# Squared-relu attention with all its matmuls in 64-row halves of the array

## The chip, the core and the metric

The kernel runs on one core of a Trainium2 chip. The metric is the time of the device in microseconds (us), as the median over runs of the whole program. The profile is of one execution more, taken by the hardware profiler.

## What is computed

```
scores = z @ z.T / S                       # per batch: S = 3072, 64 columns of z
attn   = maximum(scores, 0) ** 2
x      = u * (attn @ v)                    # D = 256; 8 batches, 24576 rows in all
logits = x @ w_gate                        # 8 experts; softmax; argmax picks one
# the first 768 rows (capacity) of each expert, in order of the rows:
out[i] = gate[i] * (maximum(x[i] @ w1[e], 0) @ w2[e])   # F = 1024; other rows are 0
```

All inputs are float32. Rows that come after an expert is full give zero, so the kernel stops the attention as soon as all eight experts are full.

## The kernel before

**Tiles.** A group is 384 rows of x (three tiles of 128), eight groups a batch. Keys come in 24 chunks of 128, two chunks a double (PAIRS = 12 doubles a group). Float32 values are split in two float16 parts, high and low; products high by high, high by low and low by high are summed in PSUM. zP holds the high part of one half of the keys on partitions 0 to 63 and the low part on 64 to 127 (the other way round for the batch's second half), zQ the same with the halves crossed. One matmul of zP by zP has high by high and low by low, one of zP by zQ the two mixed terms: scores() gives two matmuls of 384 columns for each of the two chunks (L640, L641).

**A double.** TensorE: scores of double c+3 (LEAD), then the values of double c: weigh() issues for each of three tiles and two chunks three matmuls of 256 columns (L676 high by high v, L678 high by low v, L680 low by high v), all summed over 128 keys, into one accumulator a tile (o_part). ScalarE: relu in place in PSUM (do_relu, L462), square with a scale into `attn` in SBUF (do_square, L466). VectorE: a float16 copy attn_hi (do_hi, L941) and the rest attn_lo (do_lo, L947). There are four score banks, two for even and two for odd doubles; `scores(K)` wait until the square of K-2 is done. Values wait for `lo_done`.

**Banks.** O has two banks (three tiles of 256 columns), Sc four, M two: the logits in one, the counts in the other.

**Between groups.** gate_x, at VectorE's step c=11 and before that step's do_hi, multiplies O by the factor of the batch and by u in one operation (L988 for tiles 0 and 1, L992 for tile 2). TensorE's first values of the next group wait for it (evac_done). ScalarE, at c=0, sums absolute values of the result (L503, three times), from which VectorE works out a scale; ScalarE writes high parts at c=1 (L508), VectorE low parts at its c=0 (L1041); SyncE transposes rows by DMA. TensorE does the logits (L717, 12 matmuls of 16 columns) behind tile 2 of c=3 and the counts (L725, L729, 4 matmuls) behind tile 1 of c=4. VectorE routes at its c=3 (L1086 to L1124), all of it between do_lo of the sixth double and do_hi of the seventh; GpSimd scatters the rows to their experts' places.

**Steps beside these.** The engines' programs are the same loop over groups with fixed places for side work: in the last four groups of a batch the split of the next batch's z and v (ScalarE c=6 to 9, VectorE c=7 to 9, among it z_lo_across, a copy to the other half of the partitions, L911), in groups 1 and 2 of a batch the sums of absolute v on ScalarE (L438), four a group. After double END_AT every engine reads whether all experts are full (load_end) and if so leaves. Then the experts' two layers run, in 16 rounds.

**Order.** All engines but TensorE's weight loads go strictly in the order of their programs. wait_apart is a wait on a value that is held in a register, with an increment of a spare semaphore.

## Time and profile before

| | |
|---|---|
| median of 3 runs | 867.1 us (867.08 to 867.22) |
| the profiled execution's span | 865.3 us |
| TensorE busy | 853.5 us (99%) |
| VectorE busy | 632.4 us (73%) |
| ScalarE busy | 574.7 us (66%) |
| GpSimd busy | 123.2 us (14%) |
| attention's last matmul, experts' first | 609.09 us, 609.80 us |
| granted clock of TensorE | full in the whole span |

The median is 1.8 us above the span; what lies between is around the first and the last instruction. Matmuls are pipelined and their ends are modelled: what one costs in a stream is read from start to start. A line is that of the source, L12 line 12. "<-" behind an idle time names what ended it. PE is TensorE's matmuls, PEld its weight loads, DVE VectorE, ACT ScalarE, POOL GpSimd.

### The profile page before, as it was taken

What the parts mean: (1) busy time and instruction counts of PE and PEld (TensorE: products, weight loads), DVE (VectorE), ACT (ScalarE), POOL (GpSimd) and SP (SyncE); (2) the same over time, 40 slices, a digit from 0 to 9 for tenths busy, and PEclk for the clock granted to TensorE, in tenths of its full rate; (3) what the DMA queues carried; (4) which work ended last, traced back from release to release, by engine and by line L of the source; (5) the groups of instructions that cost most, each with busy time, mean ns of one, the idle gap of its engine ahead of it and who ended that gap; (6) DMA issues with size and microseconds to landing.
All of it is one profiled execution on the core that took longest, in us unless ns stands there. A gap on an engine that the chain in (4) does not pass through costs nothing.

```text
span 865.3 us, 22736 instructions
## 1 busy us (share of the span) xinstructions
PE 853.5 (99%) x7258; PEld 683.9 (79%) x7259; DVE 632.4 (73%) x1380; ACT 574.7 (66%) x874; POOL 123.2 (14%) x121
## 2 busy tenths in 40 slices
PE   6999999999999999999999999999999999999997
PEld 5888888888888888888888888888777777777776
DVE  7976777988889878887888798687464655565531
ACT  7978786868778779777778777678434434435422
POOL 1001102101101110110110110110112121211212
PEclk9999999999999999999999999999999999999999
DMA  7922343343312633312313313731625325415101
GB/s 274 372 70 94 87 129 136 100 135 117 118 46 97 240 108 97 115 49 92 115 50 98 107 53 108 264 82 40 145 65 171 102 80 158 142 46 152 55 18 36
DMA packets 104277, 98.62 MB, mean 114 GB/s; under 512 B 67149, under 2 KB 91802, under 8 KB 103232
## 3 DMA queue, kind: packets, MB, share of 16 engines
q1 hardware_dynamic: 99360, 85.71, 32.1%
q0 software_dynamic: 4896, 12.64, 4.0%
q8 instruction: 12, 0.20, 0.1%
q14 instruction: 9, 0.07, 0.0%
HBM read 40.03 MB, written 44.93 MB: 98 GB/s over the span
## 4 chain that ended last, share of the span: by engine, by line
PE 97%; DVE 2%; issue 1%; POOL 0%; ACT 0%; POOLq 0%; DVEq 0%; ACTq 0%
PE O L676 17%; PE O L678 17%; PE O L680 17%; PE Sc L786 14%; PE Sc L640 8%; PE Sc L641 8%; PE O L809 3%; PE O L813 3%; PE O L811 3%; PE M L809 2%; PE M L813 2%; PE M L811 2%; PE M L717 1%; PE M L615 0%; DVE zQ L904 0%
## 5 line engine op out<-in xcount | busy, mean ns | idle before, releaser
L676 PE MATMUL O<-vS,attn_hi 128*128 128x256 f16 x1332 | 363.0, 273 | 0.3 <-DVE vS L930 0.3
L680 PE MATMUL O<-vS,attn_lo 128*128 128x256 f16 x1332 | 363.0, 273 | 0.0
L678 PE MATMUL O<-vS,attn_hi 128*128 128x256 f16 x1332 | 363.0, 273 | 0.0
L462 ACT ACTIVATE Sc<-Sc 128x768 f32<-128x768 f32 x224 | 178.0, 795 | 86.3 <-PE Sc L641 78.4
L947 DVE TENSOR_TENSOR attn_lo<-attn,attn_hi 128x768 f16<-128x768 f32 x223 | 213.7, 958 | 7.7
L466 ACT ACTIVATE attn<-Sc 128x768 f32<-128x768 f32 x224 | 181.7, 811 | 7.1
L676 PEld LDWEIGHTS O<-vS,attn_hi 128*128 128x128 f16 x1332 | 130.2, 98 | 27.2 <-issue 0.4
L678 PEld LDWEIGHTS O<-vS,attn_hi 128*128 128x128 f16 x1332 | 130.3, 98 | 26.6
L640 PE MATMUL Sc<-zP 128*128 (+1 forms) x450 | 146.4, 326 | 2.1 <-DVE zP L911 1.3
L641 PE MATMUL Sc<-zQ,zP 128*128 (+1 forms) x450 | 146.4, 326 | 0.0
L941 DVE CAST attn_hi<-attn 128x768 f16<-128x768 f32 x223 | 123.7, 555 | 27.4 <-ACT attn L466 26.0
L680 PEld LDWEIGHTS O<-vS,attn_lo 128*128 128x128 f16 x1332 | 130.3, 98 | 15.1
L1251 DVE SCALAR_TENSOR_TENSOR rawv<-Sc,rawv 128x768 f16<-128x768 f32 x63 | 60.1, 956 | 110.1 <-ACT rawv L571 110.1
L380 POOL DMA_INDIRECT disp<-xrow,slot x54 | 68.2, 1263 | 486.8 <-DVE slot L1123 453.2
L571 ACT ACTIVATE rawv<-Sc 128x768 f16<-128x768 f32 x63 | 51.1, 811 | 100.8 <-PE Sc L786 99.7
L786 PE MATMUL Sc<-vS,w1h 128*128 128x384 f16 x384 | 78.1, 326 | 0.0
L809 PE MATMUL O<-w2s,rawv 128*128 128x256 f16 x256 | 69.8, 273 | 0.0
L813 PE MATMUL O<-w2s,rawv 128*128 128x256 f16 x256 | 69.8, 273 | 0.0
L811 PE MATMUL O<-w2s,rawv 128*128 128x256 f16 x256 | 69.8, 273 | 0.0
L415 POOL DMA_INDIRECT out<-attn,vS x48 | 47.0, 980 | 113.6 <-ACT attn L583 99.9
L640 PEld LDWEIGHTS Sc<-zP 128*128 128x128 f16 (+1 forms) x450 | 43.9, 98 | 20.4 <-DVE zQ L925 1.5
L641 PEld LDWEIGHTS Sc<-zQ,zP 128*128 128x128 f16 (+1 forms) x450 | 44.0, 98 | 17.1
(155 smaller groups left out, 912.4 us busy)
## 6 DMA issues: line engine op xcount, KB each, us to landing
out<-empty SPq DMA_DIRECT2D x16, 1536.0 KB, 6.3
wraw<-in_moe_w SPq DMA_DIRECT2D x16, 1024.0 KB, 7.0
rawv<-in_v SPq DMA_DIRECT2D x14, 768.0 KB, 8.5
ubuf<-in_u SPq DMA_DIRECT2D x19, 384.0 KB, 3.1
disp<-vS SPq DMA_DIRECT2D x8, 774.0 KB, 9.1
rawz<-in_z SPq DMA_DIRECT2D x3, 768.0 KB, 6.0
xT<-xrow SPq DMA_TRANSPOSE x54, 2.4
disp<-xrow,slot POOLq DMA_INDIRECT x54, 2.8
```

Of the source, the lines that this page charges most:

```text
L462: act.activation(pair, pair, ACT.Relu).then_inc(s["relu_done"], 1)
L466: act.activation(attn[:, c % BUFS, :, :], Sp[:, 2 * (c % 2):2 * (c % 2) + 2, 0:GROUP], ACT.Square, scale=ROOT_C).then_inc(s["square_done"], 1)
L640: nc.tensor.matmul(to, keys, zP[:, bass.ds(qb, GROUP)], start=True, stop=False)
L641: ins = nc.tensor.matmul(to, keys, zQ[:, bass.ds(qb, GROUP)], start=False, stop=True)
L676: nc.tensor.matmul(o_part(t), hi, v[:, 0:D], start=c == 0 and j == 0 and t % 2 == 0, stop=False, skip_group_check=True)
L678: nc.tensor.matmul(o_part(t), hi, v[:, D:2 * D], start=False, stop=False, skip_group_check=True)
L680: ins = nc.tensor.matmul(o_part(t), lo, v[:, 0:D], start=False, stop=c == PAIRS - 1 and j == 1, skip_group_check=True)
L786: ins = nc.tensor.matmul(Sp[:, 2 * (p % 2) + fi, 0:GROUP], w[par][:, m, f * P:(f + 1) * P], xt[k][:, x + m, :], start=(at == 0), stop=(at ...
L809: nc.tensor.matmul(y_part(t), hi, w2s[:, par, f, 0:D], start=f == 0, stop=False, skip_group_check=True)
L811: nc.tensor.matmul(y_part(t), hi, w2s[:, par, f, D:2 * D], start=False, stop=False, skip_group_check=True)
L941: dve.tensor_copy(attn_hi[:, b, :, :].rearrange("p j n -> p (j n)"), attn[:, b, :, :].rearrange("p j n -> p (j n)")).then_inc(s["hi_done"], 1)
L947: dve.tensor_tensor(attn_lo[:, b, :, :], attn[:, b, :, :], attn_hi[:, b, :, :], ALU.subtract).then_inc(s["lo_done"], 1)
```

## The change

Every matmul of the attention phase, the logits and counts too, becomes two: one on partitions 0 to 63 of both operands, one on 64 to 127, issued one after the other and writing to different banks (helper `half`).

- **Scores.** In zP and zQ the high and the low part of a chunk's keys stand on different halves of the partitions. Three terms (high by high, high by low, low by high), each a pair: half 0 does chunk 0 of the double, half 1 chunk 1. Low by low is left out.
- **Values.** The same three matmuls as before, each in two halves of 64 keys, into two sets of banks: O has four banks. M is gone; logits and counts use score banks 2 and 3 (`beside`), and in the loop all scores use banks 0 and 1 (`score_banks`). The norms of the next batch go there too.
- **Relu** goes from PSUM into `attn`, square works in place there. `scores(K)` wait for the relu of K-1.
- **Joining the two sums.** ScalarE copies the second half's banks, scaled, into `lower` (in the memory of xT), VectorE adds the first half's, scaled (evac_done), and multiplies by u in another operation (`gated`). gate_x now comes after do_lo of step c=11. The values of the last two doubles are reordered (TURNS) so that tiles 0 and 1 end earlier. Logits and counts are summed over the halves by VectorE.
- **Queries** are copied by GpSimd into fixed buffers (q_now for the running group, q_next and k_next for the first doubles of the next); it also does z_lo_across.
- **Places.** Logits behind c=3, counts behind c=4 (all tiles), END_AT from 5 to 6, steps of norms and scales later, several small buffers shared.

The diff, cut to its core (smaller memory for tables and renamings are left out):

```diff
-        Oa = ps("O", [P, 2, 512], F32)
+        Os = ps("O", [P, 4, 512], F32)
         Sp = ps("Sc", [P, 4, 512], F32)
-        Mp = ps("M", [P, 2, 512], F32)
-
-        def o_part(t):
-            return Oa[:, t // 2, (t % 2) * D:(t % 2 + 1) * D]
-
-        M = [Mp[:, m, :] for m in range(2)]
+
+        def half(r):
+            return slice(64 * r, 64 * r + 64)
+
+        def o_part(r, t):
+            return Os[:, 2 * r + t // 2, (t % 2) * D:(t % 2 + 1) * D]
+
+        def beside(r, at, columns):
+            return Sp[:, 2 + r, at:at + columns]
+
+        both_counts = Sp[:, 2:4, COUNTS_FROM:COUNTS_FROM + (TILES + 1) * E].rearrange("p r n -> p n r")
+        both_norms = Sp[:, 2:4, 0:GROUP]
+
+        def score_banks(K):
+            return K % 2 if isinstance(K, int) else 0
...
+            def queries(to, m, ready):
+
+                at = (m & 15) * GROUP
+                for q, z16 in zip(to, (zP, zQ)):
+                    pool.tensor_copy(q[:, :], z16[:, bass.ds(at, GROUP)]).then_inc(s[ready], 1)
+
+            def keys(m):
+
+                at = (m & 8) * (S // 8)
+                for k, z16 in zip(k_next, (zP, zQ)):
+                    pool.tensor_copy(k[:, :], z16[:, bass.ds(at, SLICE * P)]).then_inc(s["k_next_ready"], 4)
+
             def body(n, end):
                 g = n & 7
                 if isinstance(n, int):
+                    pool.wait_ge(s["khi_ready"], 2)
+                    pool.wait_ge(s["klo_ready"], 2)
+                    queries(q_now, 1, "q_now_ready")
+                    keys(0)
 
                     pool.wait_ge(s["disp_filled"], 16 * (E * capacity // P // FILL_ROWS))
                     pool.sem_inc(s["row_free"], 1)
                     return
+                wait_apart(pool, s["scores_ready"], n * PAIRS + LEAD)
+                for key in ("khi_ready", "klo_ready"):
+                    wait_apart(pool, s[key], ((n + 1) & 126) + 2)
+                queries(q_next, n + 1, "q_next_ready")
+                only_if(pool, g == 7, lambda: keys(n + 1))
...
+                def keys_low_across():
+
+                    wait_apart(pool, s["q_next_ready"], n * 2)
+                    wait_apart(pool, s["k_next_ready"], ((n + 1) & 120) + 8)
+                    wait_apart(pool, s["zlo_ready"], (n & 120) + g * 2 + 2)
+                    cols = bass.ds(((n + 8) & 8) * (S // 8) + (g & 3) * (SLICE * P), SLICE * P)
+                    with pool.If(g < 6):
+                        pool.tensor_copy(zP[half(1), cols], zQ[half(0), cols]).then_inc(s["klo_ready"], 2)
+                    with pool.Else():
+                        pool.tensor_copy(zQ[half(0), cols], zP[half(1), cols]).then_inc(s["klo_ready"], 2)
+                    wait_apart(pool, s["klo_ready"], (n & 120) + g * 2 + 2)
+
                 def rest():
+                    only_if(pool, g > 3, keys_low_across)
                     only_if(pool, g == 3, reduce_maxes)
                     only_if(pool, n == 7, lambda: all_w(0))
                     only_if(pool, n == 12, lambda: all_w(1))
+                    wait_apart(pool, s["scores_ready"], n * PAIRS + PAIRS)
+                    queries(q_now, n + 1, "q_now_ready")
...
-                pair = Sp[:, 2 * (c % 2):2 * (c % 2) + 2, 0:GROUP]
-                act.activation(pair, pair, ACT.Relu).then_inc(s["relu_done"], 1)
+                at = 2 * score_banks(K)
+                act.activation(attn[:, c % BUFS, :, :], Sp[:, at:at + 2, 0:GROUP], ACT.Relu).then_inc(s["relu_done"], 1)
 
             def do_square(K, c):
                 act.wait_ge(s["relu_done"], K + 1)
-                act.activation(attn[:, c % BUFS, :, :], Sp[:, 2 * (c % 2):2 * (c % 2) + 2, 0:GROUP], ACT.Square,
-                               scale=ROOT_C).then_inc(s["square_done"], 1)
+                act.activation(attn[:, c % BUFS, :, :], attn[:, c % BUFS, :, :], ACT.Square, scale=ROOT_C
+                               ).then_inc(s["square_done"], 1)
...
+                        if not peeled and c == LOWER_AT:
+                            wait_apart(act, s["fcur_ready"], ((n - 1) & 120) + 8)
+                            act.wait_ge(s["o_ready"], n * 2 - 1)
+                            act.activation(lower[:, 0:2, :].rearrange("p t d -> p (t d)"), Os[:, 2, :], ACT.Copy,
+                                           scale=fcur[:, 0:1]).then_inc(s["lower_ready"], 1)
+                            act.wait_ge(s["o_ready"], n * 2)
+                            act.activation(lower[:, 2, :], Os[:, 3, 0:D], ACT.Copy,
+                                           scale=fcur[:, 0:1]).then_inc(s["lower_ready"], 1)
                         if not peeled and c == L1_AT:
                             for t in range(TILES):
-                                act.wait_ge(s["evac_done"], n * 2 - 1 + t // 2)
+                                act.wait_ge(s["gated"], n * 2 - 1 + t // 2)
...
-                if not (isinstance(K, int) and K < 2):
-                    if par is None:
-                        wait_apart(pe, s["square_done"], K - 1)
-                    else:
-                        pe.wait_ge(s["square_done"], K - 1)
-                qb = (n & 15) * GROUP
-                for j in range(2):
-                    at = (2 * c + j) * P
-                    kb = (n & 8) * (S // 8) + at if par is None else par * S + at
-                    keys, to = zP[:, bass.ds(kb, P)], Sp[:, 2 * (c % 2) + j, 0:GROUP]
-                    nc.tensor.matmul(to, keys, zP[:, bass.ds(qb, GROUP)], start=True, stop=False)
-                    ins = nc.tensor.matmul(to, keys, zQ[:, bass.ds(qb, GROUP)], start=False, stop=True)
+                if not isinstance(K, int):
+                    wait_apart(pe, s["relu_done"], K)
+                elif K >= 2:
+                    pe.wait_ge(s["relu_done"], K - 1)
+
+                def key_cols(z16, k_first, r):
+                    at = (2 * c + r) * P
+                    return k_first[half(r), at:at + P] if par is None else z16[half(r), par * S + at:par * S + at + P]
+
+                def query_cols(z16, q_first, q_rest, r):
+                    if isinstance(n, int):
+                        return z16[half(r), n * GROUP:(n + 1) * GROUP]
+                    return (q_first if par is None else q_rest)[half(r), :]
+
+                high_keys, low_keys = (
+                    [key_cols((zP, zQ)[x], k_next[x], r) for x, r in ((h, 0), (1 - h, 1))] for h in range(2))
+                high_queries, low_queries = (
+                    [query_cols((zP, zQ)[x], q_next[x], q_now[x], r) for x, r in ((h, 0), (1 - h, 1))] for h in range(2))
+                terms = ((high_keys, high_queries), (high_keys, low_queries), (low_keys, high_queries))
+                for at, (keys, queries) in enumerate(terms):
+                    for r in range(2):
+                        ins = nc.tensor.matmul(Sp[:, 2 * score_banks(K) + r, 0:GROUP], keys[r], queries[r],
+                                               start=at == 0, stop=at == len(terms) - 1)
...
-                        hi, lo = (a[:, c % BUFS, j, t * P:(t + 1) * P] for a in (attn_hi, attn_lo))
-                        v = vS[:, par * CHUNK + 2 * c + j, :]
-
-                        nc.tensor.matmul(o_part(t), hi, v[:, 0:D], start=c == 0 and j == 0 and t % 2 == 0,
-                                         stop=False, skip_group_check=True)
-                        nc.tensor.matmul(o_part(t), hi, v[:, D:2 * D], start=False, stop=False,
-                                         skip_group_check=True)
-                        ins = nc.tensor.matmul(o_part(t), lo, v[:, 0:D], start=False,
-                                               stop=c == PAIRS - 1 and j == 1, skip_group_check=True)
+                        first, last = c == 0 and j == 0 and t % 2 == 0, c == PAIRS - 1 and j == 1
+                        for at, (weights, low_values) in enumerate(((attn_hi, 0), (attn_hi, 1), (attn_lo, 0))):
+                            for r in range(2):
+                                ins = nc.tensor.matmul(
+                                    o_part(r, t), weights[half(r), c % BUFS, j, t * P:(t + 1) * P],
+                                    vS[half(r), par * CHUNK + 2 * c + j, low_values * D:(low_values + 1) * D],
+                                    start=first and at == 0, stop=last and at == 2, skip_group_check=True)
...
+                            if not peeled and c == 0:
+                                wait_apart(pe, s["q_now_ready"], n * 2)
...
+                                    wait_apart(pe, s["q_next_ready"], n * 2)
+                                    wait_apart(pe, s["k_next_ready"], ((n + 1) & 120) + 8)
                             scores(K0 + c + LEAD, n + 1, c + LEAD - PAIRS, 0 if peeled else None)
 
-                        pe.wait_ge(s["lo_done"], K0 + c + 1)
+                        wait_apart(pe, s["lo_done"], K0 + c + 1)
                         if peeled:
                             pe.wait_ge(s["split_ready"], (2 * c + 1) // UNIT + 1)
-                        for t in range(TILES):
+                        for of, t in TURNS.get(c, [(c, t) for t in range(TILES)]):
                             if c == 0 and not peeled and t != 1:
 
-                                pe.wait_ge(s["evac_done"], n * 2 - 1 + t // 2)
-                            ins = weigh(c, t)
-                            if c == PAIRS - 1 and t:
+                                wait_apart(pe, s["evac_done"], n * 2 - 1 + t // 2)
+                            ins = weigh(of, t)
+                            if of == PAIRS - 1 and t:
                                 ins.then_inc(s["o_ready"], 1)
...
+                        if not peeled and c == LOGITS_AT:
...
+                            for k in range(TILES):
+                                for at, (h, m) in enumerate((h, m) for h in range(2) for m in range(DC)):
+                                    for r in range(2):
+                                        ins = nc.tensor.matmul(beside(r, k * 2 * E, 2 * E),
+                                                               xT[half(r), k, h * DC + m, :], wgs[half(r), m, :],
+                                                               start=at == 0, stop=at == 2 * DC - 1,
...
+                        if not peeled and c == COUNTS_AT:
+                            wait_apart(pe, s["onehot_ready"], n)
+                            for r in range(2):
+                                nc.tensor.matmul(beside(r, COUNTS_FROM, (TILES + 1) * E), before[half(r), :],
+                                                 onehot[half(r), :, :].rearrange("p t e -> p (t e)"),
+                                                 start=True, stop=False, skip_group_check=True)
+                            for k in range(TILES):
+                                for r in range(2):
+                                    ins = nc.tensor.matmul(
+                                        beside(r, COUNTS_FROM + (k + 1) * E, (TILES - k) * E), ones[half(r), :],
+                                        onehot[half(r), k:k + 1, :].to_broadcast([64, TILES - k, E]),
+                                        start=False, stop=k == TILES - 1, skip_group_check=True)
+                            ins.then_inc(s["counts_ready"], 1)
...
+                for k, tiles in enumerate((slice(0, 2), slice(2, 3))):
+                    dve.wait_ge(s["lower_ready"], n * 2 - 1 + k)
+                    dve.scalar_tensor_tensor(out=lower[:, tiles, :].rearrange("p t d -> p (t d)"),
+                                             in0=Os[:, 0, :] if k == 0 else Os[:, 1, 0:D], scalar=fcur[:, 0:1],
+                                             in1=lower[:, tiles, :].rearrange("p t d -> p (t d)"),
+                                             op0=ALU.mult, op1=ALU.add).then_inc(s["evac_done"], 1)
+                    dve.wait_ge(s["evac_done"], n * 2 - 1 + k)
+                    dve.tensor_tensor(ubuf[:, tiles, :], lower[:, tiles, :], ubuf[:, tiles, :], ALU.mult
+                                      ).then_inc(s["gated"], 1)
...
-                        if c == PAIRS - 1:
-
-                            gate_x(n + 1)
                         do_hi(K0 + c + 2, c + 2)
                         do_lo(K0 + c + 2, c + 2)
+                        if c == PAIRS - 1:
+                            gate_x(n + 1)
...
-                            counts = M[1][:, 0:TILES * E].rearrange("p (t e) -> p t e", t=TILES)
+                            route(dve.tensor_reduce(csum[:, :], both_counts, AX.X, ALU.add))
+                            counts = csum[:, 0:TILES * E].rearrange("p (t e) -> p t e", t=TILES)
...
+TURNS = {PAIRS - 2: [(PAIRS - 2, 0), (PAIRS - 2, 1)],
+         PAIRS - 1: [(PAIRS - 1, 0), (PAIRS - 1, 1), (PAIRS - 2, 2), (PAIRS - 1, 2)]}
...
-LOGITS_AT = (3, 2)
-COUNTS_AT = (4, 1)
+LOGITS_AT = 3
+COUNTS_AT = 4
...
-END_AT = 5
+END_AT = 6
```

## Rows read from the trace of the kernel before

**Rows 1.** The page: busy us, share of the span and instructions of each engine
```profile
PE 853.5 (99%) x7258; PEld 683.9 (79%) x7259; DVE 632.4 (73%) x1380; ACT 574.7 (66%) x874; POOL 123.2 (14%) x121
```

**Rows 2.** The stretch view of one group's length: busy us of each engine
```profile
56.70:88.57 31.87, 31.87 (x283) 26.09 (x281) 23.91 (x59) 25.37 (x43) 3.77 (x3) 1.00 0.29 89
```

**Rows 3.** The page's groups of instructions: busy us, mean ns of one | idle before
```profile
L676 PE MATMUL O<-vS,attn_hi 128*128 128x256 f16 x1332 | 363.0, 273 | 0.3 <-DVE vS L930 0.3
```

**Rows 4.** The timeline at a boundary: start us, us, engine, line
```profile
400.05 0.33 PE L641 MATMUL Sc<-zQ,zP 128*128 x1
...
400.21 0.27 PE L676 MATMUL O<-vS,attn_hi 128*128 128x256 f16 x1
400.21 0.10 PEld L678 LDWEIGHTS O<-vS,attn_hi 128*128 128x128 f16 x1
...
402.17 0.33 PE L640 MATMUL Sc<-zP 128*128 x1
...
402.82 0.27 PE L676 MATMUL O<-vS,attn_hi 128*128 128x256 f16 x1
```

**Rows 5.** The timeline of TensorE at the start
```profile
13.79 2.40 PE L647 MATMUL O<-ones,identh 128*128 128x128 f16 x40
```

**Rows 6.** The timeline of TensorE around logits and counts of the same group
```profile
412.63 0.45 PE L717 MATMUL M<-wgs,xT 128*128 128x16 f16 x12
412.94 0.32 PE L640 MATMUL Sc<-zP 128*128 x1
...
414.89 0.18 PE L725 MATMUL M<-onehot,before 128*128 128x32 f16 x1
...
415.00 0.27 PE L676 MATMUL O<-vS,attn_hi 128*128 128x256 f16 x1
```

**Rows 7.** The timeline of ScalarE behind the same boundary
```profile
400.41 0.80 ACT L462 ACTIVATE Sc<-Sc 128x768 f32<-128x768 f32 x1 [0.98 <-PE Sc L641]
401.23 0.81 ACT L466 ACTIVATE attn<-Sc 128x768 f32<-128x768 f32 x1
402.50 0.42 ACT L503 ACTIVATE xrow<-ubuf 128x256 f16<-128x256 f32 x1 [0.46 <-DVE ubuf L988]
...
403.72 0.79 ACT L462 ACTIVATE Sc<-Sc 128x768 f32<-128x768 f32 x1
...
406.44 0.80 ACT L462 ACTIVATE Sc<-Sc 128x768 f32<-128x768 f32 x1
```

**Rows 8.** The groups of VectorE and ScalarE by form
```profile
L947 DVE TENSOR_TENSOR attn_lo<-attn,attn_hi 128x768 f16<-128x768 f32 x223 | 213.7, 958 | 7.7
...
L992 DVE SCALAR_TENSOR_TENSOR ubuf<-O,fcur,ubuf 128x256 f32<-128x256 f32 x18 | 8.5, 474 | 0.0
...
L571 ACT ACTIVATE rawv<-Sc 128x768 f16<-128x768 f32 x63 | 51.1, 811 | 100.8 <-PE Sc L786 99.7
...
L583 ACT ACTIVATE attn<-O,fac 128x256 f32<-128x256 f32 x32 | 15.1, 473 | 18.4 <-PE O L813 18.4
...
L587 ACT ACTIVATE rawv<-Sc 128x384 f16<-128x384 f32 x1 | 0.5, 491 | 4.4 <-PE Sc L786 4.4
```

**Rows 9.** The timeline of VectorE in the same group
```profile
401.72 0.75 DVE L988 SCALAR_TENSOR_TENSOR ubuf<-O,fcur,ubuf 128x512 f32<-128x512 f32 x1 [2.45 <-PE O L680]
...
413.12 0.21 DVE L1086 TENSOR_REDUCE logit<-M 128x24 f32<-128x48 f32 x1 [0.61 <-PE M L717]
...
415.18 0.16 DVE L1112 TENSOR_TENSOR base<-base,M 128x8 f32<-128x8 f32 x1
...
416.57 0.55 DVE L941 CAST attn_hi<-attn 128x768 f16<-128x768 f32 x1
```

**Rows 10.** The timeline of ScalarE in group 1, with sums of v
```profile
72.28 0.80 ACT L462 ACTIVATE Sc<-Sc 128x768 f32<-128x768 f32 x1 [0.34 <-ACT xT L438]
...
75.50 0.80 ACT L462 ACTIVATE Sc<-Sc 128x768 f32<-128x768 f32 x1 [0.61 <-ACT xT L438]
```

**Rows 11.** The groups of GpSimd by form
```profile
L364 POOL MEMSET vS<- 128x1542 f32 x1 | 1.4, 1383 | 0.3 <-POOLq L1348 0.3
```

## What the change is predicted to do

> **What bounds the kernel now.** I read the page's busy times first, then one group in the stretch view, then the timelines. TensorE is busy 853.5 of 865.3 us [rows 1], and what it waits for lies at the start. So the change is worth what it takes off TensorE's stream, less what it makes TensorE wait. A group lasts 31.87 us; in it VectorE is busy 23.9 us and ScalarE 25.4 us [rows 2]. Neither is the bound on average, but both work in strict order, so what counts is which wait ends last at each place. 1332 matmuls at L676 are 222 doubles of six [rows 3]: the flat group 0, seventeen full ones and six doubles of group 18, with 18 boundaries and 18 routings. The pace inside a double: four score matmuls from 402.17 to 402.82, 0.163 us each; eighteen value matmuls from 400.21 to 402.17, 0.109 each; 2.61 us in all [rows 4]. The durations 0.33 and 0.27 beside them are modelled ends, not occupancy.
>
> **Scores.** Two matmuls a key chunk, four a double, become three pairs of half matmuls. If the two of a pair run together, a double's scores cost 3 x 0.163 = 0.49 in place of 0.65. Values stay at 18 x 0.109 = 1.96, now as 18 pairs. A double falls to 2.45 us: 222 x 0.163 = **-36.2 us**. This rests on a pair costing what one matmul costs. Bounds: 40 matmuls of 128 columns take 2.40 us, the tail of the last (0.23 less its own step) included, so 0.0556 each [rows 5]; against 0.109 at 256 columns that is 0.0533 per 128 columns and 0.0023 fixed. If the other half hides the fixed part, 21 x 222 x 0.0023 = 10.7 us go besides; if both halves' parts stand one behind the other, 10.7 us come on top. I take the middle, since nothing in the trace speaks for either end. The second bound is the sequencer, which must hand over a load and a matmul every 0.054 us: the trace shows 0.0556 kept up over 40 [rows 5] and 0.026 for twelve in a row [rows 6]; the middle lies between these too.
>
> The trace has the load for L678 starting at 400.21 together with the matmul of L676, on the same rows of the array [rows 4]. The Trainium skill (TensorE: Matmul & The Clock Gate, The mechanism) says that a load overlaps matmuls in flight only when its row group differs; by that rule each half would stand still for its own next load, by the row it does not. The same section's span model adds about 4 ns for the second tile of a pair; by that, an estimate, 21 x 222 x 4 ns = 19 us would come on top of the sum.
>
> **Small matmuls.** Logits go from 12 to 24; twelve took 412.63 to 412.94, so +0.31. Counts go from 4 to 8; four took 414.89 to 415.00, so +0.11 [rows 6]. They lie on TensorE and nothing hides them: 18 x 0.42 = **+7.6 us** (nothing, if the halves' loads run side by side; this pace looks like one of instructions, so I take the full price). END_AT 6 instead of 5 gives a seventh double of group 18: **+2.5 us**. Fixed query buffers, the closing matmuls, norms and start-up change by tenths: nothing. The last phase is not touched.
>
> **The boundary.** Times from V, the start of the values of c=11 (400.21 before). The last score matmul began at 400.05 and ended at V+0.17, relu began at V+0.20, square 0.82 after it [rows 4, 7]. With TURNS, tiles 0 and 1 of the old group end after twelve pairs, V + 11 x 0.109 + 0.27 = V+1.47. ScalarE is still in its square then. (Relu into SBUF and square out of it keep their length: 768 columns from PSUM to SBUF took 0.811 [rows 8].) Its new copy of the lower half's sum starts at V+1.78. A scaled copy of 256 columns took 0.473; 384 columns more of one operation took 0.811 - 0.491 = 0.32 [rows 8], so 256 more make 0.69: V+2.47. VectorE's fused operation of 512 columns took 0.75 [rows 9], to V+3.25. TensorE wants the bank at V + 24 x 0.109 + 0.49 = V+3.11 and restarts about 0.1 after the signal (a load's recorded length [rows 4]): **0.24 lost**.
> VectorE then multiplies by u, now an operation of its own: 768 columns at L947 took 0.958; 256 columns are 0.751 - 0.474 = 0.28 [rows 8, 9], so 512 make 0.68, to V+3.96. The second bank takes 0.47 and 0.41 more, less what neighbours overlap: V+4.82. ScalarE's last absolute sum waits for this (the three took 402.50 to 403.72, 0.40 each [rows 7]), so its relu of the next double starts at V+5.25 and ends at V+6.05. Here stands the new wait: in the loop all scores use one pair of banks, and scores(K) wait for relu(K-1), where they waited for square(K-2). TensorE wants c=1's scores at V+3.35+1.96 = V+5.31 and starts them at V+6.17: **0.86 lost**. The 36 value matmuls of c=1, whose inputs are long there, are queued behind that wait. Relu, square and three row copies took 2.72 (403.72 to 406.44 [rows 7]), 0.03 more with square from SBUF: the next relu runs from V+8.00 to V+8.82; TensorE wants c=2's scores at V+8.62 and goes on at V+8.94: **0.32 lost**. Then ScalarE has caught up. 1.42 us a boundary, 18 times: **+25.6 us**. Bounds: nothing, if each of the scaled durations is short; 1.9 each, if a copy on GpSimd holds VectorE up as well.
>
> **The routing.** L is the start of the logits (412.63). VectorE read them at L+0.49 and was ready for the counts at L+2.55 (415.18) [rows 6, 9]; now L+0.80 and L+2.86. But the counts move from behind tile 1 to behind all of c=4: L + 0.62 + 2.45 + 0.22 and a tail of 0.17, L+3.46. The new addition over the halves takes 0.24, the old steps 1.39 (415.18 to 416.57 [rows 9]), so the cast of the seventh double starts at L+5.1 and its attn_lo, 0.58 and 0.96 later, ends at L+6.63. TensorE wants it in c=6 at L + 0.64 + 2.45 + 0.22 + 2.45 + 0.49 = L+6.25 and starts at L+6.75: 0.5 x 18 = **+9.0 us**. Bounds: nothing (it had 0.75 us to spare before) to 1 us each.
>
> **The sums of v.** In five groups ScalarE has one of these in each of c=6 to 9, and relu then follows relu by 3.2 us (72.28 to 75.50) [rows 10], against TensorE's 2.45. Relu(K-1) may be late by 1.96 - 0.17 - 0.85 - 0.1 = 0.84 us. The first two are covered by that and by the stall of c=6, the last two lose about 0.47 each: 5 x 0.95 = **+4.8 us**. Bounds nothing to 8.
>
> **GpSimd.** It gets four copies of 384 columns a group, and in four groups of a batch the crossing of the low keys, which VectorE did. q_now is wanted 2.4 us behind a boundary, and the keys cross near the end of the group before. The only plain row of its speed is a fill of 1542 elements in 1.38 us [rows 11]: 0.35 us a copy, 0.7 for the crossing. Several times that is still hidden; past about five times TensorE would wait at every boundary. I put nothing, and 0 to 9 us (0.5 a group) in the range for VectorE being held up.
>
> **Sum.** -36.2 + 7.6 + 2.5 + 25.6 + 9.0 + 4.8 = +13.3, a span of 878.6 from 865.3. The median of the runs stands 1.8 above that span: **880 us**.
>
> **Rivals.**
> (a) Faster: the stalls are mostly covered. The chain at the boundary has eight links, four of them scaled from other shapes. With none of the 39.4 us lost it is 841, with half 861, likeliest 850; it decides below 24 us of stalls. For it: the removed matmuls lay on the bounding engine, and a hidden fixed part would give 10.7. Against: ScalarE's order is strict, and the new wait is for its latest relu. Chance 0.28.
> (b) The forecast, 869 to 890: 0.48.
> (c) Slower still: a pair pays both fixed parts or the sequencer's 0.0556, 10 us, and GpSimd's copies cost up to 9: 890 to 902. 0.14.
> (d) It does not do what it says: the halves take turns, 222 x (18 x 0.109 + 2 x 0.163) = +508 us, near 1380. Or each pair stands still for a load, at least 21 x 222 x 0.026 = +121 us, about 1000; the load under its neighbour's matmul [rows 4] speaks against that. 0.04 together. The second is what the skill's rule on loads, told above, would make of the pairs.
> (e) Within 0.2%, which is about what a measurement of this kernel can tell from no change: 0.06.
>
> **Range.** 846 to 902 leaves out (d), the edge of (c) and the best of (a). Slower 0.66, same 0.06, faster 0.28. The likeliest case's own range is 869 to 890.
>
> **What would show it.** Value matmuls starting in pairs 0.109 apart and score pairs 0.163 apart: the saving. TensorE waiting for ScalarE's relu once or twice behind each boundary, 1.4 us in all, groups of 32 us or more, and a wait for attn_lo in c=6: the stalls. Groups of 30 us or less would refute the stalls; a pair of 0.12 or more would refute the saving.

## The result and the profile after

The changed kernel takes 906.42 us (median of 4 runs, 905.95 to 907.31) where the kernel before takes 867.12 in the same comparison: ratio 1.0454, 95% interval 1.0439 to 1.0469. It is slower, as forecast, but by 39 us in place of 13, and 4 us above the range's end of 902. The profiled execution has a span of 904.5 us.

The page of the kernel after: busy times, DMA queue for instructions, shares of the chain that ended last, and two groups (busy, mean ns of one | idle before).
```profile
PE 845.7 (93%) x12045; PEld 712.4 (79%) x12046; DVE 671.7 (74%) x1427; ACT 609.5 (67%) x914; POOL 193.2 (21%) x207
...
q8 instruction: 27, 0.44, 0.2%
...
PE 59%; ACT 13%; issue 12%; DVE 10%; DVEq 2%; ACTq 1%; DMA 1%; POOL 1%; POOLq 0%; SPq 0%
...
L757 PE MATMUL O<-vS,attn_hi 64*128 64x256 f16 x5352 | 455.7, 270 | 10.4 <-DVE attn_lo L1033 8.0
...
L721 PE MATMUL Sc<-q_now,zP 64*128 64x384 f16 x480 | 107.3, 323 | 27.3 <-POOL q_now L392 10.0
```
The same two lines of the page of the kernel before, which [rows 1] leaves out:
```profile
q8 instruction: 12, 0.20, 0.1%
...
PE 97%; DVE 2%; issue 1%; POOL 0%; ACT 0%; POOLq 0%; DVEq 0%; ACTq 0%
```
TensorE was the chain (97%); now 41% of the chain lies elsewhere. Its stream did become shorter. TensorE's timeline of the kernel after, the double with logits and the one with counts of group 1:
```profile
61.26 0.47 PE L801 MATMUL Sc<-wgs,xT 64*128 64x16 f16 x24
61.56 0.32 PE L721 MATMUL Sc<-q_now,zP 64*128 64x384 f16 x1
...
62.05 0.40 PE L757 MATMUL O<-vS,attn_hi 64*128 64x256 f16 x4
...
64.01 0.20 PE L809 MATMUL Sc<-onehot,before 64*128 64x32 f16 x2
...
64.12 0.32 PE L721 MATMUL Sc<-q_now,zP 64*128 64x384 f16 x1
...
64.60 0.40 PE L757 MATMUL O<-vS,attn_hi 64*128 64x256 f16 x4
```
Scores take 0.49 (61.56 to 62.05), the 36 value halves 1.96 (62.05 to 64.01, 0.109 a pair): 2.45 for a double, where it was 2.61 [rows 4]. What TensorE waits for in the kernel after (us in total, times, longest):
```profile
PE Sc L721 <- ACT attn L515: 12.9, 26, 1.0
PE Sc L721 <- POOL q_now L392: 10.0, 7, 2.5
PE Sc L721 <- issue: 8.3, 15, 4.5
PE O L757 <- DVE attn_lo L1033: 8.0, 18, 0.6
PE O L728 <- DVE ones L947: 4.5, 1, 4.5
PE O L728 <- issue: 4.1, 1, 4.1
```
Only the 4.5 us for `ones`, at the start, was there before. These waits count idle time behind modelled ends, so they come out shorter than the loss. For the whole loss I took every double of groups 1 to 18: from the start of its scores to the start of the next double's, less 2.45 (0.30 more where the logits stand, 0.11 where the counts do, 0.65 moved from c=10 to c=11 for the order of tiles). What remains is lost, by place, in us over all groups; the last column says how much of the sum is a low granted clock (0.50 where it is 1.00 else). The kernel before loses 2.6 in all by the same reckoning, at 2.61 a double, with no low clock in these groups.

| | c=0, 1 | c=2 to 5 | c=6 | c=7 | c=8 | c=9, 10 | c=11 to the next scores | sum | of it low clock |
|---|---|---|---|---|---|---|---|---|---|
| predicted | 25.6 | 0 | 9.0 | 0 | \* | \* | 0 | 39.4 | 0 |
| after | 20.5 | 0.1 | 14.6 | 2.5 | 9.1 | 2.5 | 17.8 | 67.2 | 3.4 |
| e1 queries first | 30.1 | 0.3 | 14.4 | 5.0 | 8.9 | 2.5 | 7.5 | 68.7 | 1.7 |
| e2 routing split | 20.3 | 0.5 | 3.4 | 4.7 | 9.7 | 2.5 | 19.4 | 60.5 | 3.4 |
| e3 sums after relu | 4.3 | 36.5 | 14.7 | 4.9 | 10.5 | 2.5 | 16.4 | 89.8 | 5.1 |
| e5 places moved | 30.5 | 1.6 | 3.1 | 1.9 | 8.0 | 1.6 | 10.8 | 57.4 | 12.0 |
| e6 sums kept | 35.3 | 0.3 | 6.6 | 0.2 | 8.1 | 0.4 | 7.7 | 58.5 | 1.7 |
| e9 copies by DMA | 30.7 | 0.0 | 14.5 | 5.0 | 9.0 | 2.5 | 14.0 | 75.7 | 8.5 |
| e10 DMA and places | 11.8 | 3.1 | 2.6 | 1.7 | 11.9 | 0.6 | 47.7 | 79.5 | 15.4 |
| e13 one wait | 20.7 | 0.4 | 14.7 | 5.7 | 5.5 | 3.5 | 17.4 | 67.9 | 3.4 |

\* The 4.8 us for the sums of v lay at c=7 to 10. (e4 has another pace, and in e14 too many matmul records are missing for this reckoning.)

Behind the groups the time differs once more: between the attention's last values and the experts' first matmul TensorE stands 4.1 us in the kernel after, e5 and e6 (4.0 to 4.3), and 0.8 us in e1, e2, e3, e9, e10 and e13; the last phase then takes 257.7 us in the kernel after and 255.5 in those six. So 5.5 us of their difference from the kernel after come from a place that none of their edits touches, and have to be set against each measured time below.

### The profile page after: what moved, and what is told of

Its sections match the earlier page's. It is cut to its first block, busy times and chain, and to the rows that moved or that the text cites. A ratio compares the mean times of both kernels' runs of the same rounds, so it can differ in the third digit from the quotient of the medians.

```text
span 904.5 us, 33240 instructions
## 1 busy us (share of the span) xinstructions
PE 845.7 (93%) x12045; PEld 712.4 (79%) x12046; DVE 671.7 (74%) x1427; ACT 609.5 (67%) x914; POOL 193.2 (21%) x207
## 3 DMA queue, kind: packets, MB, share of 16 engines
q1 hardware_dynamic: 99360, 85.71, 30.5%
## 4 chain that ended last, share of the span: by engine, by line
PE 59%; ACT 13%; issue 12%; DVE 10%; DVEq 2%; ACTq 1%; DMA 1%; POOL 1%; POOLq 0%; SPq 0%
PE O L757 23%; PE Sc L873 14%; PE Sc L721 7%; ACT attn L515 6%; PE O L896 5%; PE O L898 5%; PE O L900 5%; DVE attn_hi L1027 3%; ACT xrow L569 2%; DVE ubuf L1080 2%; ACT xrow L564 2%; DVE xT L1075 2%; DVE attn_lo L1033 1%; DMA rawv<-in_v 1%; ACT xT L556 1%
## 5 line engine op out<-in xcount | busy, mean ns | idle before, releaser
L757 PE MATMUL O<-vS,attn_hi 64*128 64x256 f16 x5352 | 455.7, 270 | 10.4 <-DVE attn_lo L1033 8.0
L757 PE MATMUL O<-vS,attn_lo 64*128 64x256 f16 x2676 | 386.7, 270 | 0.0
L757 PEld LDWEIGHTS O<-vS,attn_hi 64*128 64x128 f16 x5352 | 296.3, 94 | 40.9 <-issue 21.2
L515 ACT ACTIVATE attn<-Sc 128x768 f32<-128x768 f32 x225 | 181.0, 804 | 64.3 <-PE Sc L721 51.9
L519 ACT ACTIVATE attn<-attn 128x768 f32<-128x768 f32 x225 | 190.0, 844 | 7.1
L757 PEld LDWEIGHTS O<-vS,attn_lo 64*128 64x128 f16 x2676 | 152.1, 94 | 0.4
L1027 DVE CAST attn_hi<-attn 128x768 f16<-128x768 f32 x224 | 130.2, 581 | 25.6 <-ACT attn L519 22.2
L721 PE MATMUL Sc<-q_now,zP 64*128 64x384 f16 x480 | 107.3, 323 | 27.3 <-POOL q_now L392 10.0
L896 PE MATMUL O<-w2s,rawv 128*128 128x256 f16 x384 | 104.7, 273 | 0.0
L900 PE MATMUL O<-w2s,rawv 128*128 128x256 f16 x384 | 104.7, 273 | 0.0
L898 PE MATMUL O<-w2s,rawv 128*128 128x256 f16 x384 | 104.7, 273 | 0.0
L721 PE MATMUL Sc<-q_now,zQ 64*128 64x384 f16 x480 | 102.2, 326 | 0.0
L721 PEld LDWEIGHTS Sc<-q_now,zP 64*128 64x128 f16 x480 | 38.3, 93 | 45.2 <-issue 45.2
L873 PEld LDWEIGHTS Sc<-vS,w1h 128*128 128x128 f16 x384 | 37.6, 98 | 21.0
```

Source lines behind the costliest of these rows:

```text
L515: act.activation(attn[:, c % BUFS, :, :], Sp[:, at:at + 2, 0:GROUP], ACT.Relu).then_inc(s["relu_done"], 1)
L519: act.activation(attn[:, c % BUFS, :, :], attn[:, c % BUFS, :, :], ACT.Square, scale=ROOT_C).then_inc(s["square_done"], 1)
L721: ins = nc.tensor.matmul(Sp[:, 2 * score_banks(K) + r, 0:GROUP], keys[r], queries[r], start=at == 0, stop=at == len(terms) - 1)
L757: ins = nc.tensor.matmul(o_part(r, t), weights[half(r), c % BUFS, j, t * P:(t + 1) * P], vS[half(r), par * CHUNK + 2 * c + j, low_values * ...
L873: ins = nc.tensor.matmul(Sp[:, 2 * (p % 2) + fi, 0:GROUP], w[par][:, m, f * P:(f + 1) * P], xt[k][:, x + m, :], start=(at == 0), stop=(at ...
L896: nc.tensor.matmul(y_part(t), hi, w2s[:, par, f, 0:D], start=f == 0, stop=False, skip_group_check=True)
```

## The experiments

Ratios are against the kernel before, in the same comparison, with the 95% interval.

**e1: the queries ahead of the crossing keys.** In GpSimd's rest of a group:
```diff
-                    only_if(pool, g > 3, keys_low_across)
...
                     queries(q_now, n + 1, "q_now_ready")
+                    only_if(pool, g > 3, keys_low_across)
```


> Edit: GpSimd copies the running group's queries (q_now) before it carries the low keys across, not after. Theory (waits in strict order): behind groups 4 to 7 and 12 to 15 TensorE stands 0.9 to 2.7 us for q_now, 17.8 us at that place in all, 4.3 of it something else at one boundary. Taken away, these boundaries get back the relu loss of the others (0.86 instead of 0.2 to 0.4 at c=0), so about 8 us are won: 898 us. Rival (the place is bound by instruction fetch or by ScalarE): below 2 us won, 905. The one long stop of 4.5 us behind group 15 stays in both.

Measured 902.82, ratio 1.0415 (1.0397 to 1.0432). The loss behind the groups falls from 17.8 to 7.5, of which 4.3 stand behind group 15 alone, and 9.6 come back at c=0, 1, where TensorE, now earlier, waits for the relu: 18.7 us for L515 in place of 12.9. So the wait for q_now is GpSimd's order, and it had been covering the boundary's own stop in the same groups. By place e1 loses as much as the kernel after (68.7 and 67.2); the 3.6 us by which it is faster are the stop at the attention's end. What TensorE waits for is GpSimd's chain, here in the kernel after, at the boundary of groups 7 and 8 (timeline; VectorE, GpSimd and TensorE):
```profile
279.96 1.02 DVE L990 SCALAR_TENSOR_TENSOR zP<-rawz,zscale,zQ  x1 [0.37 <-issue]
...
281.84 1.40 POOL L440 COPY zQ<-zP  x1 [9.58 <-DVE zP L990]
...
282.48 1.18 DVE L1027 CAST attn_hi<-attn 128x768 f16<-128x768 f32 x1
...
283.71 1.18 POOL L429 PARTITION_ALL_REDUCE wamx<-wmx  x1 [0.47 <-POOL zQ L440]
...
284.76 0.57 POOL L392 COPY q_now<-zP 128x384 f16 x1
...
286.17 0.47 PE L721 MATMUL Sc<-q_now,zP 64*128 64x384 f16 x1 [2.48 <-POOL q_now L392]
```
The crossing waits for z's low half, which VectorE writes until 280.98; the copies that TensorE wants first are queued behind it.

**e2: the routing over one double more.**
```diff
-ROUTE_AT = (3, 3, 3)
+ROUTE_AT = (3, 3, 4)
```


> Edit: VectorE does the part of the routing that needs the counts after attn_lo of the seventh double, not before it. Theory: the 0.6 us that TensorE stands in every c=6 for attn_lo go, 10.8 us in 18 groups, less what ScalarE's relu then costs in c=7 and c=8 (it has less time to catch up, 0.1 to 0.3 a group): 897 us. Rival (c=6 is held by the relu chain): 904 to 906.

Measured 893.46, ratio 1.0300 (1.0283 to 1.0317). c=6 falls from 14.6 to 3.4, 11.2 us, and 4 to 5 come back (2.2 at c=7, 0.6 at c=8, 1.6 behind the groups): 6.7 us by place for one constant. The rest of the 13 us is the 5.5 at the attention's end. It is the only one of these edits taken alone that lowers the sum by place.

**e3: the absolute sums behind the next relu.**
```diff
-L1_AT = 0
+L1_AT = 1
-RSCALE_AT = 0
+RSCALE_AT = 1
-ROWS_HI_AT = 1
-ROWS_LO_AT = 0
+ROWS_HI_AT = 2
+ROWS_LO_AT = 1
```


> Edit: the absolute sums, the row scale and the row copies each one step later, so that relu of the next double comes before them on ScalarE. Theory: the 0.85 and 0.32 us lost at c=0 and c=1 behind each boundary go (19.3 us in all), the transposes start 0.9 us later and are just in time for the logits: 889 us, 0 to 0.3 a group given back at c=3. Rival (the transposes are late): the loss moves to c=3 and the time stays above 900.

Measured 923.79, ratio 1.0660 (1.0642 to 1.0678): the rival held. The relu's stop is gone (c=0, 1: 20.5 to 4.3), which shows what it was made of, but x is transposed a double later and the logits at c=3 wait for that. TensorE's waits in e3:
```profile
PE Sc L801 <- DMA xT<-xrow: 29.8, 18, 2.1
```

**e4: values over the full 128 rows, the rest in halves.** One matmul for each pair of value halves, one sum, one fused evacuation, as in the kernel before:
```diff
-                            for r in range(2):
-                                ins = nc.tensor.matmul(
-                                    o_part(r, t), weights[half(r), c % BUFS, j, t * P:(t + 1) * P],
+                            ins = nc.tensor.matmul(
+                                o_part(0, t), weights[:, c % BUFS, j, t * P:(t + 1) * P],
```


> Edit: values in full matmuls of 128 rows into one set of banks and evacuated in one fused operation, scores, logits and counts in halves as in the change. So the array changes between halves and whole twice a double. Theory (a change of form costs nothing that a stream of matmuls doesn't hide): the boundary's chain is the short one of the kernel before, 19 us won, 886 us. Rival (at each change the array runs empty): one tail of 0.166 us (0.273 less 0.107) twice in 222 doubles, +74 us, 960; 0.05 each would give +22, 908.

Measured 902.06, ratio 1.0398 (1.0381 to 1.0416). TensorE's timeline in e4:
```profile
96.64 0.32 PE L713 MATMUL Sc<-q_now,zP 64*128 64x384 f16 x1
96.90 0.39 PE L748 MATMUL O<-vS,attn_hi 128*128 128x256 f16 x2
...
98.76 0.27 PE L748 MATMUL O<-vS,attn_lo 128*128 128x256 f16 x1
98.97 0.19 PE L800 MATMUL Sc<-onehot,before 64*128 64x32 f16 x2
...
99.08 0.32 PE L713 MATMUL Sc<-q_now,zP 64*128 64x384 f16 x1
```
The last score pair starts at 96.64 and the values 0.26 later, where a pair's pace is 0.163. The last value matmul starts at 98.76 and the counts, in halves, 0.21 later, where the pace is 0.109. So a change between half and full matmuls costs 0.10 us. There are two in a double: 222 x 0.2 = 44 us, more than the 36 that the halves save. This gives the second half of the change, the values in halves, its reason: they save nothing themselves, but keep the form. The theory (886 us) failed, and the rival held at about twice its milder price (0.05 a change). It also shows the price of the values' halves: without the second evacuation e4 has no stop for the relu at the boundary, and with its shorter program (25080 executed instructions on all engines against 33240) no stop of that size behind group 15.

**e5 and e6: the three orders together.** e5 has e1, e2, e3, the logits one double later so that the transposes have their time, v's and z's splits at other doubles:
```diff
-LOGITS_AT = 3
-COUNTS_AT = 4
+LOGITS_AT = 4
+COUNTS_AT = 5
-ZHI_AT = (8, 9)
-ZLO_AT = 9
-VHI_AT = (6, 7)
-VLO_AT = (7, 8)
+ZHI_AT = (6, 8)
+ZLO_AT = 7
+VHI_AT = (3, 4)
+VLO_AT = (8, 9)
```
e6 is e5 with the absolute sums and the logits left where they were.

> Edit: q_now first on GpSimd, the counts' part of the routing behind attn_lo, absolute sums and row copies one step later, and now the logits, counts and routing one double later too (END_AT 7), so that the transposes have 2.45 us more; the splits and the sums of v on ScalarE spread over c=3 to 9. Theory (every stop is a wait in strict order, and each can be moved away): of the 66 us that TensorE stands in groups 1 to 18 some 45 go: 4 us left at c=0 and c=1, 3 at c=6, 6 at c=7 to 9, 6 at the boundary with the stop of 4.3 us behind group 15, and one more double costs 2.5: 862 us, faster than the kernel before (867). Rival (each wait that goes is taken up by the next one in line, as with the transposes in the run with later sums): above 875.

> Edit: as the run with all places moved, but the absolute sums, row copies, logits, counts and END_AT stay where the change has them. Theory: the relu stop of 0.85 and 0.32 us behind each boundary stays (20 us), the rest goes: 880 us. Against the run with all places moved it should be slower by 18 us; if it isn't, the later sums are not worth their place.

Measured 894.49, ratio 1.0297 (1.0273 to 1.0320), and 896.44, ratio 1.0333 (1.0315 to 1.0350). e5's rival held. e6 missed its 880, and it lies 2 us above e5 in place of the 18 expected, less than e5's own runs differ (890.6 to 898.4): the later sums are not worth their place. TensorE's waits in e5:
```profile
PE O L757 <- DVE xT L1075: 17.4, 11, 2.1
PE Sc L721 <- issue: 8.7, 18, 4.3
...
PE Sc L721 <- ACT attn L515: 4.0, 10, 1.2
```
In groups 2, 3, 10, 11 and 17, which have no splits, e5 loses 1.0 to 1.4 us a group: there the order is right. In groups 5 to 8 and 12 to 15 the relu's stop has turned into some 2.1 us of waiting for VectorE's evacuation. I take that for v's low halves, which VectorE has at c=8 and 9, and GpSimd's copies, which stretch its operations (the cast of 0.56 took 1.18 beside the crossing copy, in the fence under e1); e10, which moves both, loses nothing there in groups 3 to 8. These waits cost more than themselves: in groups 6 and 12 to 15 the clock was granted at 0.50 for 3.4 us behind them. In the profiled execution 12.0 of the 57.4 us are that low clock, and of e5's runs the one with the highest mean clock (0.990) is the fastest, 890.6, that with the lowest (0.984) the slowest, 898.4.

**e8: GpSimd's copies alone, in the kernel before.** Four copies of 384 columns a group into buffers that nobody reads.
```diff
+                for q, z16 in zip(dummy, (zP, zQ)):
+                    pool.tensor_copy(q[:, :], z16[:, bass.ds((n & 15) * GROUP, GROUP)]
+                                     ).then_inc(s["dummy_ready"], 1)
```


> Edit: the kernel before, with four copies of 384 columns a group on GpSimd into buffers that nobody reads, at the places of the change. Theory (before, the copies fall into VectorE's slack): attn_hi and attn_lo are held up by up to 1 us where they meet a copy, TensorE doesn't wait, 867 to 868 us. Rival (the lock of the two engines costs time by itself): 0.5 us a group, 876.

Measured 867.28, ratio 0.9999 (0.9989 to 1.0009). The copies took 0.64 and 0.75 us each on average there and VectorE's attn_lo rose from 958 [rows 8] to 967 ns. So copies that nobody waits for cost nothing where VectorE has slack, and the rival, a lock that costs time by itself, failed.

**e9: GpSimd's query copies as DMAs** on SyncE's queue, same buffers, same readers:
```diff
-                    pool.tensor_copy(q[:, :], z16[:, bass.ds(at, GROUP)]).then_inc(s[ready], 1)
+                    sp.dma_start(q[:, :], z16[:, bass.ds(at, GROUP)]).then_inc(s[ready], 16)
```


> Of the kernel after, one part alone is moved: the two pairs of query copies a group (384 columns each) are DMAs on SyncE's queue instead of GpSimd's copies; same buffers, same readers. Theory (the wait for q_now is GpSimd's serial work, its crossing copies and its meetings with VectorE, and no property of the halves): the waits behind groups 4 to 7 and 12 to 15, 17.8 us in all of which 4.3 is instruction fetch, go, 13.5 us; the rest stays: 893 us. Rival (as in e1, TensorE that comes earlier only finds VectorE later): about 11 of the 13.5 come back as the evacuation's wait at the boundary, 902 us or more. Rival (a DMA is issued too late or lands too late): TensorE waits for q_now by a DMA at every boundary, 910 us or more.

Measured 909.45, ratio 1.0486 (1.0469 to 1.0504), slower than the kernel after; the first rival held and the second in two groups. The waits behind groups 4 to 7 and 12 to 14 are gone (0.1 to 0.3 us). But 10.2 us come back at the boundary, 5.8 for the relu and the evacuation and 4.4 of low clock (0.50 behind the stops of groups 8, 15 and 16), and behind groups 8 and 16 the DMA stands behind the loads of the next v on SyncE's queue, 3.2 and 3.6 us.

**e10 and e14: everything known taken away together.** e10 is e9's DMAs, the crossing of the keys by DMA as well, e5's order, v's low halves at c=6 and 7 and z's at c=8. e14 in addition issues the q_now copy before SyncE waits for the scatter and for v, and gives TensorE one wait before c=9, as e13. Of e10, against e5 (ZHI_AT goes from (6, 8) to (6, 7) besides):
```diff
-ZLO_AT = 7
-VLO_AT = (8, 9)
+ZLO_AT = 8
+VLO_AT = (6, 7)
```


> The kernel after with three things together: the query copies and the copy of the keys' low halves across are DMAs on SyncE's queue; the routing is split over three doubles and the boundary's work behind the evacuation is one double later (as in e5); and VectorE's splits of v are at c=6 and 7 and of z at c=8, so that nothing of theirs lies in the four doubles before a boundary. Theory (what e5 still lost at the boundary, 28.7 us, is VectorE that is late with work placed at c=8 and 9 and stretched by GpSimd's copies): the boundary's loss falls below 5 us, the small waits for queries (3 us) go, the fetch stops (4.5 and 4.3) and 8 us at c=8 stay: 864 us, a shade faster than the kernel before. Rival (VectorE is late because its load is too high whatever the places): over 880 us, with TensorE waiting for VectorE in groups 4 to 7 and 12 to 15.

> e10 mended: SyncE issues the q_now copy before it waits for the routing's scatter and for v, the first keys are copied by DMA too, and TensorE has one register wait before c=9. Theory (the stops are a sum of known ones: e10's 47.7 us behind the groups were DMAs issued too late): behind the groups only the fetch stop of some 5 us is left, 43 us less; the boundary's 10.5 falls to about 5 as no group starts late; c=8 from 12 to 7: 917 - 43 - 5 - 5 = 864 us, within 0.5% of the kernel before. Rival (a further cause takes their place: VectorE, busy for over 28 of 32 us, is late once TensorE is not): over 880 us, with waits for VectorE named.

e10 measured 917.27, ratio 1.0580 (1.0537 to 1.0624); e14 883.66, ratio 1.0180 (1.0164 to 1.0195), the fastest version with halves of these runs and still 16 us behind the kernel before. In e10 TensorE waits 38.5 us, 15 times, for a q_now copy. The waits of e14:
```profile
PE Sc L728 <- issue: 11.8, 12, 7.7
PE O L764 <- DVE xT L1080: 6.6, 9, 1.2
...
PE Sc L878 <- SPq L391: 3.3, 1, 3.3
```
For e10 neither the theory nor the rival came true. The theory's half on VectorE held (groups 3 to 8 lose nothing for it at c=0), but SyncE waited for the routing's scatter, a double later than before, ahead of each q_now copy. e14 mends that: 34 us less, and the stops are then mostly known ones in sum. It misses the 864 expected by 20, and its rival (over 880, with waits for VectorE named) held. Left are the stop behind group 15, now 7.7 us, 6.6 us of evacuation, 3.3 us at the start of the last phase (its first rows are now fetched behind e14's new waits on SyncE) and the rest in tenths. A version that beats the kernel before was not found.

**e13: one register wait in place of four on TensorE before c=9's scores.**
```diff
-                                    wait_keys(((n + 1) & 120) + 6)
                                     wait_apart(pe, s["q_next_ready"], n * 2)
-                                    wait_apart(pe, s["k_next_ready"], ((n + 1) & 120) + 8)
```


> The kernel after with one wait against a register instead of four on TensorE before the scores of c=9 (GpSimd copies the keys ahead of the queries and waits for the keys itself, so that q_next's count stands for all). Theory (the stop there is TensorE's own sequencer going through eleven register, semaphore and branch instructions in a row; e11 showed about 0.1 us each where nothing covers them): the issue wait of 0.26 us in 14 groups goes, and of the 9 us at c=8 some 5 remain or fewer: 902 us. Rival (it is the relu that frees the bank, as at the boundary): the same 9 us stand there with ScalarE named, 906 us.

Measured 901.06, ratio 1.0384 (1.0370 to 1.0398). TensorE's waits in e13, to be read beside those of the kernel after:
```profile
PE Sc L723 <- issue: 5.1, 4, 4.1
...
PE O L730 <- issue: 0.8, 1, 0.8
```
The issue waits fall from 15 to 4, and c=8 from 9.1 to 5.5, so the run of register waits was the stop there. But 3.2 us appear at c=7, and by place nothing is won. e1, e2, e3 and e9, whose edits are others, have the same 5 us at c=7; why is open. The 5.4 us that the kernel did gain are the 5.5 at the attention's end, which the edit doesn't touch. That the time is within 1 us of the 902 expected is luck.

**e7 and e11: a longer TensorE program in the kernel before**, 40 instructions more a double. e7's were register moves:
```diff
+                        if not peeled:
+                            for _ in range(40):
+                                pe.reg_mov(pad, 0)
```


> Edit: the kernel before, with 40 moves of a spare register in each of TensorE's doubles of the loop, so that its program is about as long as that of the change; the moves are 35 to 40 ns each on the sequencer, 1.5 of the 2.6 us of a double, and should hide under the matmuls. Theory (the stop of 4.3 us behind group 15 and the one of 4 us behind the attention are a program fetched again because the loop no longer stays in the sequencer's memory): both stops appear, 8 us together, 873 to 877 us, with instruction packets in the trace at those two places. Rival (they come from waits of the new layout): no such stops, 867 to 868.

Measured 867.55, ratio 1.0002, with 22736 executed instructions, as before: the moves are not in the program that ran, and e7 tells nothing. e11 has `pe.sem_inc(s["passed"], 1)` in their place.

> The kernel before with 40 semaphore increments more per double on TensorE's queue (9,000 executed instructions more, 31,900 in all, near the 33,200 of the kernel after; nobody waits for them). Theory (the stops of 4.65 us behind group 15 and of 4.1 us at the attention's end are the instruction fetch of a longer TensorE program): more instruction packets than 12 and such stops appear, 875 us. Rival (the stops have another cause in the changed kernel): no stop, 867 us. Rival (the increments hold up TensorE's sequencer): every double is longer by the same amount, over 880 us.

Measured 1837.71, ratio 2.1194 (2.1151 to 2.1237): the last rival held. TensorE's timeline in e11 between two doubles:
```profile
412.02 0.53 PE L641 MATMUL Sc<-zQ,zP 128*128 x1
414.17 0.27 PE L676 MATMUL O<-vS,attn_hi 128*128 128x256 f16 x1 [1.62 <-issue]
```
In the trace the 40 increments of this double start 0.15 us apart (408.10 to 414.06), 6.0 us in all, where the whole double took 2.61 before: that is what holds TensorE up, with a mean granted clock of 0.78 besides. But e11 also has what it was made for. The branch at the end of the loop over pairs of batches, which TensorE's sequencer takes behind group 15 and again when the loop ends, in the kernel before, in e11 and in the kernel after (count, shortest, median and longest in ns, first and last start in us):
```profile
L753 PEldq COMPARE_BRANCH  x2: 78/142/207, 527.9 to 609.4; - x2
...
L756 PEldq COMPARE_BRANCH  x2: 78/1708/3339, 1355.0 to 1576.4; - x2
...
L840 PEldq COMPARE_BRANCH  x2: 85/1920/3756, 551.1 to 646.4; - x2
```
It takes 0.21 us behind group 15 in the kernel before and 3.34 in e11, which differs from it by the increments alone. So a longer TensorE program is enough for this stop, and its first rival, a cause in the changed kernel's waits, failed. e11 has 23 instruction packets in place of 12.

**e12: both halves of each value pair on rows 0 to 63.** The output leaves out the values' rows 64 to 127 and counts the others twice.
```diff
-                                    o_part(r, t), weights[half(r), c % BUFS, j, t * P:(t + 1) * P],
-                                    vS[half(r), par * CHUNK + 2 * c + j, low_values * D:(low_values + 1) * D],
+                                    o_part(r, t), weights[half(0), c % BUFS, j, t * P:(t + 1) * P],
+                                    vS[half(0), par * CHUNK + 2 * c + j, low_values * D:(low_values + 1) * D],
```


> The kernel after with both matmuls of every value pair on the rows 0 to 63 (the output leaves out the values' rows 64 to 127 and counts the others twice); the scores keep their two halves. It measures what the pairs save. Theory (a pair's two matmuls run beside each other only because their rows differ): a double's 18 value pairs take 36 x 0.109 = 3.9 us instead of 1.96, so 228 doubles x 1.96 = 447 us more, some 1350 us, less what waits they cover. Rival (the pair's pace of 0.109 has nothing to do with which half it is on): 906 us.

One run: 1702.91 us. Two stretches of e12 (TensorE busy and its matmuls, then PEld, VectorE, ScalarE, GpSimd, granted clock, DMA share, GB/s) and its timeline:
```profile
200.00:300.00 100.00, 100.00 (x516) 67.08 (x515) 25.64 (x60) 27.22 (x44) 5.70 (x7) 0.50 0.09 28
600.00:700.00 100.00, 100.00 (x1011) 83.27 (x1009) 56.05 (x130) 50.94 (x76) 13.36 (x16) 1.00 0.28 91
```
```profile
401.14 1.06 PE L757 MATMUL O<-vS,attn_hi 64*128 64x256 f16 x4
...
402.42 1.06 PE L757 MATMUL O<-vS,attn_hi 64*128 64x256 f16 x4
...
410.81 0.60 PE L757 MATMUL O<-vS,attn_hi 64*128 64x256 f16 x4
...
411.47 0.60 PE L757 MATMUL O<-vS,attn_hi 64*128 64x256 f16 x4
```
Six halves take 0.66 us where the clock is 1.00 (410.81 to 411.47), 0.109 each: one half alone costs what a pair costs, so two halves on different rows run beside each other and two on the same rows don't. That is the saving's mechanism, shown on the values. The 1703 us are more than the 1350 expected for two reasons. The output is another, so the experts fill later and the attention runs 235 doubles in place of 223, by my estimate 12 x 4.41 = 53 us. And the clock is granted at 0.50 (1.2 of 2.4 GHz) for 389 us from 21.4 and for 382 us from 1065.9, where a stop of 3.7 us ends, while TensorE is busy without a gap for hundreds of microseconds; a half then costs 0.213 (401.14 to 402.42), and 771 us at half the clock cost 386. Against that, the waits of the kernel after are covered: TensorE is busy 99% of the span. Between the two, for 655 us, the same stream has 1.00; what decides between them is open. In the kernel after, with the halves side by side, the clock is 0.992 in the mean.

## Why the prediction was wrong

By its own terms, in us of the span; the part in waits is from the table of places.

| step | predicted | found |
|---|---|---|
| scores in pairs | -36.2 | -36.2 (0.49 a double) |
| small matmuls | +7.6 | 0 |
| seventh double | +2.5 | +2.5 (8028 value halves are 223 doubles) |
| boundary (c=0, 1) | +25.6 | +20.5, of it 3.0 low clock |
| routing (c=6) | +9.0 | +14.6 |
| sums of v (c=7 to 10) | +4.8 | +14.1 |
| GpSimd, q_now | 0 | +13.5 |
| stops in issue behind group 15 and at the end | 0 | +4.3 +4.1 |
| low clock after the latter | 0 | +2.2 |
| waits of the kernel before | 0 | -2.6 |
| sum | +13.3 | +37.0 |

The span rose by 39.2; 2.2 us are not placed.

**Right: what a pair costs.** Pairs start 0.109 and 0.163 apart, neither bound came true, and e12 shows the mechanism. The rule of the Trainium skill on loads (TensorE: Matmul & The Clock Gate, The mechanism), by which a half would stand still for its own next load, does not hold here: 36 halves took 1.96 us, no more than 18 full matmuls. The same section also lets a load for the background weight buffer run ahead; with that the trace agrees. Its 4 ns for the second tile don't show in the pace.

**Right: the boundary's mechanism.** The timeline of the kernel after, groups 2 to 3, the lines that the working named:
```profile
117.01 0.75 DVE L1075 SCALAR_TENSOR_TENSOR xT<-O,fcur,xT 128x512 f32<-128x512 f32 x1 [0.82 <-ACT xT L556]
...
117.37 0.32 PE L721 MATMUL Sc<-q_now,zP 64*128 64x384 f16 x1
...
120.72 0.32 PE L721 MATMUL Sc<-q_now,zP 64*128 64x384 f16 x1 [0.68 <-ACT attn L515]
...
123.49 0.32 PE L721 MATMUL Sc<-q_now,zP 64*128 64x384 f16 x1
```
c=0's scores, c=1's and c=2's start 3.35 and 2.77 apart; the forecast had them at V+2.62 (24 x 0.109), V+6.17 and V+8.94, 3.55 and 2.77 apart. The first step is 0.2 shorter because the evacuation was not late (0.24 predicted, 0 here); less 2.45 a double the stops are 0.90 and 0.32, where 0.86 and 0.32 were worked out for the relu. Over the groups it fits less well: the double of c=0 loses 0.81 to 1.59 us in the ten groups before which TensorE has no such long wait, and 0.2 to 0.4 in six of the others, where the wait for q_now covers it. In groups 8 and 16 it loses 1.6 and 1.3, and there it is the clock, granted at 0.50 from 286.0 to 289.5 and from 555.7 to 559.1, behind the stops of 2.5 and 4.5 us. Nor is it always the worked-out size: in e1, where no wait for q_now covers it, groups 4 to 8 and 12 to 15 lose 1.2 to 2.5 us at c=0. The forecast worked out one boundary, that before group 12, and took it for all eighteen.

**Wrong: GpSimd at nothing.** This is the largest term that the sum left out, 13.5 us, more than the 4 by which the time missed the range. The prices were twice to three times my estimate (the copies 0.62 to 0.98 us in the mean, single ones 0.50 to 1.32, where I had 0.35; the crossing 1.40 where I had 0.7), and I wrote that several times the price stays hidden. I had counted the slack from the end of the group's last scores to the next group's first and not followed the queue: the crossing waits for VectorE's z_lo, the copies stand behind it, and in group 7 a reduction of 1.18 us as well. That is the question of what is queued behind a wait, asked at ScalarE and TensorE and not at GpSimd. e1 shows it is the order. It shows too that the term can't be taken by itself: boundary and GpSimd together were 25.6 predicted and 34.0 found, and with the order mended they are still 33.3 (30.1 and 3.2), since the boundary's own stop takes the place. So what failed is the joint reckoning of the place, and not GpSimd's price alone.

**Wrong: small matmuls at +7.6.** 24 halves take 0.30 (61.26 to 61.56) where twelve took 0.31 [rows 6]. The halves run beside each other there too; what sets that pace was not tested.

**Too small: c=6 and c=7 to 10.** c=6 waits 0.6 for attn_lo as worked out (0.5), and the relu after it 0.2 more, that I had left out. From c=7 to c=10 the five groups with sums of v lose 7.1 us, 1.4 each, where the forecast has 0.95; its own figures don't give that either, since four steps of 3.2 us against 2.45, less 0.84 and the 0.5 of c=6, leave 1.7. The other 7.0 us are in the groups without them: 0.4 to 0.7 at c=8 in each, and 1.2 at c=7 of group 8. The run of register waits, which the sum costed at nothing as "fixed query buffers", is 3.6 of them (e13).

**Not foreseen: stops in issue.** Behind group 15 and at the attention's end, where the kernel before has none; with the low clock after the second they make 10.6 us. By this table the time would lie inside the range without them. The second, in the kernel after:
```profile
641.94 0.50 PE L830 MATMUL O<-vS,attn_hi 64*128 64x256 f16 x6
646.52 0.28 PE L728 MATMUL O<-ones,before 128*128 128x128 f16 x1 [4.08 <-issue]
646.80 1.44 PE L873 MATMUL Sc<-x,w1h 128*128 128x384 f16 x4
```
After it four matmuls take 1.44 where the kernel before has 0.81: the granted clock is 0.72 in the mean of 640 to 650, after TensorE stood idle, and from this first matmul to the end it is 257.7 us (904.5 less 646.8) in place of 255.5. Each of the stops is one branch of TensorE's sequencer: L840, shown under e11, takes 3.76 us behind group 15, and at the end it is this one, in the kernel after and in e1:
```profile
L849 PEldq COMPARE_BRANCH  x2: 77/1840/3603, 283.0 to 642.6; - x2
...
L849 PEldq COMPARE_BRANCH  x2: 77/208/338, 284.1 to 644.2; - x2
```
A packet of the instruction queue starts inside every such branch (at 552.6 and 643.6 in the kernel after); in the kernel before no such packet moves between 299 and 617. I take the stops for the fetch of a program that is now too long to be kept. For the one behind group 15 e11 shows that the length is the cause. It stands at 3.3 to 3.9 us in every version with the values in halves (4.7 in e10 and 6.9 in e14), and neither e4 nor the kernel before has it. The one at the end goes with the count of packets, 4.0 to 4.3 us with 27 (after, e5, e6) and 0.8 with 26 (e1, e2, e3, e9, e10, e13, e14). Length alone doesn't decide it: e1's edit touches only GpSimd's program, and its branch takes 0.34. What does is open.

**Why no single edit brought the gain back.** Each group has several waits that end within a microsecond or two of each other: GpSimd's q_now, the relu behind the evacuation, VectorE's evacuation. Taking one away shows the next (e1 and e9: 10 us come back at the boundary; e5: the relu's stop becomes VectorE's). Of e2's 11.2 us 4 to 5 came back. And a wait costs more than its length when the clock falls behind it: 12.0 us in e5, 15.4 in e10, 3.4 in the kernel after and none in the kernel before. With all of them moved (e14) 23 of the 39 us are won.

## What to carry to other kernels

In these streams a matmul that fills half the array costs what one on the full array does, and two on different rows cost one; but keep a stream in one form, since each change of form costs 0.1 us. When an engine gets work that it did not have, write down its queue, item by item, up to the item that the bounding engine wants: the price of one item says little. And where several waits end close together, judge an edit by what is late next, and expect the gain only when the last of them is gone. Before an edit is credited with its gain, compare the places that it doesn't touch: here 5.5 us came and went at the attention's end.

## What the runs showed of the hardware

- Half and full matmuls in turn cost about 0.10 us a change (e4: 0.26 where 0.163 is the pace, 0.21 where 0.109 is).
- With halves on the same rows the clock was granted at 0.50 for 389 and 382 us although TensorE had no gap, and at 1.00 for the 655 us between (e12); with halves side by side it is 0.992 in the mean, with 3.4 us or more at 0.50 behind some stops of 2.5 us and longer (after).
- Semaphore increments on TensorE's queue start 0.15 us apart (e11), and waits against a register come with several such instructions (e13).
- A longer TensorE program makes one branch at a loop's end take 3.3 us in place of 0.2, with an instruction packet of 16 KB inside it (e11 against before).
- A GpSimd copy of 128x384 takes 0.50 us at the least and up to 1.32 beside VectorE, whose cast of 0.56 took 1.18 beside a GpSimd copy. The Trainium skill (SBUF — State Buffer, SBUF: two separate sides) calls their common port pair an exclusive lock; the trace agrees roughly: of the 0.76 us in which that cast and the copy overlap, the cast lost 0.62 and the copy nothing (1.40, as the others).
- As DMAs, the same copies take SyncE's queue 0.5 to 1.6 us each to issue and stand behind whatever that queue waits for (e9, e10).
